# Denominator's sum moved from VectorE to GpSimd, and the column sums of w_out made in two lots

## What is computed

```python
for t in range(S):                                   # 4 batches, 8 heads, 768 steps, head_dim 48
    state = alpha[:, :, t, :, None] * state + einsum('bhd,bhe->bhde', k[:, :, t], v[:, :, t])
    y[:, :, t] = einsum('bhd,bhde->bhe', q[:, :, t], state)
x = y as 3072 tokens x 384

h = x @ w_in                                         # 384 -> 2048
P = a[0] + a[1]*h + a[2]*h*h + a[3]*h*h*h
Q = 1.0 + abs(b[0])*abs(h) + abs(b[1])*h*h
x2 = (P / (Q + 1e-06)) @ w_out                       # 2048 -> 384

h = x2 @ w_in2                                       # 384 -> 1024
solu = h * softmax(h)
ln = (solu - mean(solu)) / sqrt(var(solu) + 1e-06) * g_ln
out = ln @ w_out2                                    # 1024 -> 384
```

## Time and profile before

| what | us |
|---|---|
| median of 3 runs | 802.56 |
| lowest and highest | 801.42, 802.93 |
| the profiled execution, device time | 799.91 |
| its span, first to last instruction | 798.1 |
| PE busy | 773.5 (97%) |
| PEld busy | 720.8 (90%) |
| DVE busy | 688.1 (86%) |
| ACT busy | 593.4 (74%) |
| POOL busy | 303.9 (38%) |
| chain that ended last: PE, DVE, ACT | 68%, 14%, 9% |

### The profile page before, as it was taken

The page is one execution under the profiler, slowest core; times in us unless marked ns, Lnnn a source line. Parts: engine busy times, 40 slices in busy tenths (PEclk is TensorE's granted clock), DMA queues, the critical chain, the costliest instruction groups (busy, mean ns, idle before and its releaser), DMA issues.

```text
span 798.1 us, 16327 instructions
## 1 busy us (share of the span) xinstructions
PE 773.5 (97%) x5406; PEld 720.8 (90%) x5406; DVE 688.1 (86%) x1251; ACT 593.4 (74%) x1214; POOL 303.9 (38%) x405
## 2 busy tenths in 40 slices
PE   7999999799899999999999999999999999999998
PEld 6777778698799999999999999999999999999988
DVE  6999999799998898889888988898889888988854
ACT  6777778688877786778677867787778777877743
POOL 4999998122223232323232323232323232323211
PEclk9999999999999999999999999999999999999999
DMA  8999999200100010001000000000000000000000
GB/s 190 220 244 261 240 248 255 66 1 1 31 1 1 10 41 11 1 12 39 10 0 14 35 10 0 21 28 10 0 35 14 10 0 10 11 11 6 5 21 30
DMA packets 93542, 42.96 MB, mean 54 GB/s; under 512 B 80632, under 2 KB 90432, under 8 KB 93504
## 3 DMA queue, kind: packets, MB, share of 16 engines
q1 hardware_dynamic: 88944, 28.92, 15.2%
q0 software_dynamic: 4560, 13.57, 5.8%
HBM read 33.04 MB, written 9.44 MB: 53 GB/s over the span
## 4 chain that ended last, share of the span: by engine, by line
PE 68%; DVE 14%; ACT 9%; issue 4%; DMA 2%; SPq 1%; ACTq 0%; DVEq 0%; POOL 0%
PE h_ps L1172 18%; PE acc_ps L1198 18%; PE y_ps L1154 12%; PE z_ps L1216 12%; PE chunks_ring L337 2%; DVE work L1416 2%; PE z_ps L1226 2%; DVE rec L1408 2%; DVE den L1404 2%; DMA chunks_kin<-in_k_dram 2%; ACT rec L1305 1%; ACT g_hi L1295 1%; DVE chunks_kp L624 1%; DVE chunks_err L617 1%; DVE chunks_rec L620 1%
## 5 line engine op out<-in xcount | busy, mean ns | idle before, releaser
L1355 POOL TENSOR_TENSOR g_lo<-work,g_hi 128x384 fp32r<-128x384 f32 x128 | 130.8, 1022 | 401.5 <-ACT g_hi L1295 401.5
L1172 PE MATMUL h_ps<-x,w 128*128 (+1 forms) x1143 | 224.8, 340 | 6.0 <-DVE work L1426 4.4
L1198 PE MATMUL acc_ps<-g_hi,w 128*128 128x384 f32 x768 | 218.3, 338 | 2.3 <-POOL g_lo L1355 2.3
L1172 PEld LDWEIGHTS h_ps<-x,w 128*128 128x128 f32 x1143 | 200.5, 188 | 12.3 <-DVE work L1426 8.5
L1198 PEld LDWEIGHTS acc_ps<-g_hi,w 128*128 128x128 f32 x768 | 141.2, 188 | 2.8 <-POOL g_lo L1355 2.8
L1267 ACT ACTIVATE h<-h_ps 128x384 f32<-128x384 f32 x128 | 61.7, 482 | 98.9 <-PE h_ps L1172 98.8
L1198 PE MATMUL acc_ps<-g_lo,w 128*128 128x384 f32 x384 | 129.7, 338 | 0.0
L1421 DVE SCALAR_TENSOR_TENSOR den<-h,ncoef,den 128x384 f32<-128x384 f32 x128 | 78.6, 614 | 39.9 <-ACT den L1270 39.0
L1216 PE MATMUL z_ps<-w,x 128*128 128x512 f32 x396 | 99.9, 397 | 2.4 <-DVE lnT L1438 2.4
L1154 PE MATMUL y_ps<-w,lnT 128*128 128x384 f32 x528 | 99.9, 338 | 0.0
L1295 ACT ACTIVATE g_hi<-work 128x384 fp32r<-128x384 f32 x128 | 68.1, 532 | 38.2 <-DVE work L1416 35.0
(11 more groups left out here) (162 smaller groups left out, 1120.8 us busy)
## 6 DMA issues: line engine op xcount, KB each, us to landing
chunks_kin<-in_k_dram SPq DMA_DIRECT2D x32, 144.0 KB, 3.7
chunks_vin<-in_v_dram SPq DMA_DIRECT2D x16, 288.0 KB, 4.7
wstage<-in_moe_w_in_dram POOLq DMA_DIRECT2D x9, 512.0 KB, 5.0
attention_out<-solu SPq DMA_DIRECT2D x64, 72.0 KB, 3.1
out_dram<-ysb SPq DMA_DIRECT2D x24, 192.0 KB, 1.8
work<-in_alpha_dram SPq DMA_DIRECT2D x30, 144.0 KB, 4.3
chunks_qin<-in_q_dram POOLq DMA_DIRECT2D x28, 144.0 KB, 4.8
x<-attention_out SPq DMA_DIRECT2D x7, 576.0 KB, 3.9
```

Source lines behind the costliest of these rows:

```text
L1172: mm = nc.tensor.matmul(h_ps[:, s % 2, 0:TT], w1[:, wz, kc, s * P:(s + 1) * P], xs[:, xz, kc, :], start=(n == 0), stop=(n == 3 * KC - 1))
L1198: mm = nc.tensor.matmul(acc_ps[:, dc, 0:TT], w2[:, wz, f, dc * P:(dc + 1) * P], rhs, start=(f == 0 and n == 0), stop=(f == FC1 - 1 and n = ...
L1355: nc.gpsimd.tensor_tensor(g_lo[:, 1 - o, :], gate[:, 1 - o, :], g_hi[:, 1 - o, :].bitcast(F32), ALU.subtract).then_inc(glo_done, 1)
```

## The change

The sum of the denominator becomes a plain addition of two tiles and moves to GpSimd, at the head of its step. For that ACT's Square is scaled by the square root of |b1|, so that `h2` holds |b1| h*h. The root is made before the loop: ACT takes the absolute value in the attention's pair 14, GpSimd raises it to 0.5 behind the last weights and signals `coef_ready`, which is now what GpSimd waits for before the main loop. DVE's operation in each step goes, with its wait for `hw_ready`, and so do DVE's max (L1451) and wait ahead of the loop. The 16 matmuls of the column sums leave steps 2 to 9 of tile 0 and stand, eight and eight, behind h in steps 1 and 2.

```diff
@@ -515,6 +519,10 @@
                                      accum_out=seen[:, 3, bass.ds(n, 1)]).then_inc(ksq_seen, 1)
             if stage1(n):
                 squares_of_v(n, p, i + o)
+            if i_is(n, NPAIR - 2):
+
+                act.wait_ge(over.coef_loaded, 32)
+                nc.scalar.activation(over.b1_size, over.b1, ACT.Abs).then_inc(over.b1_size_done, 1)
             if i_is(n, NPAIR - 1):
 
                 act.wait_ge(x0_loaded, 16)
...
@@ -721,7 +729,7 @@
             nc.gpsimd.tensor_tensor(onehot[:], ident[:, 0:HB], ident[:, HB:P], ALU.add).then_inc(zeroed, 1)
             pool.wait_ge(zeroed, 5)
         pool.wait_ge(w_lo, over.w_pieces)
-        pool.wait_ge(neg_done, 1)
+        pool.wait_ge(coef_ready, 1)
         pool.sem_inc(joined, 1)
 
     def sync(sp):
...
@@ -863,6 +871,8 @@
         ident = sb("ident", [P, P])
         coef = sb("coef", [P, 6])
         ncoef = sb("ncoef", [P, 6])
+        half = sb("half", [P, 1])
+        b1_size = sb("b1_size", [P, 1])
         gln = sb("gln", [P, FC2])
         fits = sb("fits", [1, 1], mybir.dt.int32)
         work = sb("work", [P, 2, 2, TT])
...
@@ -878,6 +888,7 @@
         wstage = sb("wstage", [P, 2, 1024], F32, phase_a)
         coef_loaded = sem("coef_loaded")
         neg_done = sem("neg_done")
+        b1_size_done = sem("b1_size_done")
         coef_ready = sem("coef_ready")
         w_loaded = [sem(f"w_loaded{j}") for j in range(2)]
         w_scaled = sem("w_scaled")
...
@@ -950,13 +961,17 @@
                     nc.gpsimd.dma_start(stage(j + 2), pieces[j + 2][0]).then_inc(w_loaded[j % 2], 16)
             pool.wait_ge(coef_loaded, 32)
             nc.gpsimd.tensor_scalar(ncoef[:], coef[:], -1.0, None, ALU.mult).then_inc(neg_done, 1)
+            nc.gpsimd.memset(half[:], 0.5).then_inc(neg_done, 1)
+            pool.wait_ge(neg_done, 2)
+            pool.wait_ge(b1_size_done, 1)
+            nc.gpsimd.tensor_tensor(ncoef[:, 5:6], b1_size[:], half[:], ALU.pow).then_inc(coef_ready, 1)
 
 
         over = Handover(work[:], x, w1, h_ps, att_stored, x0_loaded, xhi_done, x_ready, h_ready, att_copied, judged, g_ln, gln[:], gln_ready,
-                        len(list(weight_pieces())))
+                        len(list(weight_pieces())), coef[:, 5:6], b1_size[:], coef_loaded, b1_size_done)
         with phase_a:
             chunks = attention_by_chunks(nc, ctx, q, k, v, alpha, scratch, ident, fits, prepare_weights, homes, w_lo, solu[:], over)
-        scan, joined = attention_by_scan(nc, ctx, q, k, v, alpha, scratch, ident, fits[:], w_lo, neg_done, solu[:], over)
+        scan, joined = attention_by_scan(nc, ctx, q, k, v, alpha, scratch, ident, fits[:], w_lo, coef_ready, solu[:], over)
 
 
         x2 = sb("x2", [P, 2, KC, TT], F32R)
...
@@ -1173,15 +1188,15 @@
                                                           xs[:, xz, kc, :], start=(n == 0), stop=(n == 3 * KC - 1))
                                     n += 1
                             mm.then_inc(h_ready, 1)
-                        if i_is(i, 0) and 2 <= s < FC2 + 2:
-
-                            fc = s - 2
-                            if fc == 0:
+                        if i_is(i, 0) and s in (1, 2):
+
+                            if s == 1:
                                 pe.wait_ge(share_ready, 1)
-                            for z in (HI, LO):
-                                mm = nc.tensor.matmul(y_ps[:, 0:DM], share, w4[:, z, fc, :], start=(fc == 0 and z == HI),
-                                                      stop=(fc == FC2 - 1 and z == LO))
-                            if fc == FC2 - 1:
+                            for fc in range(FC2 // 2 * (s - 1), FC2 // 2 * s):
+                                for z in (HI, LO):
+                                    mm = nc.tensor.matmul(y_ps[:, 0:DM], share, w4[:, z, fc, :], start=(fc == 0 and z == HI),
+                                                          stop=(fc == FC2 - 1 and z == LO))
+                            if s == 2:
                                 mm.then_inc(means_summed, 1)
                         if s == 3:
                             last_product(i, s)
...
@@ -1264,7 +1279,7 @@
                             act.wait_ge(h_ready, g + 1)
                             if not (i_is(i, 0) and s == 0):
                                 act.wait_ge(den_ready, g)
-                            nc.scalar.activation(h2[:], hp, ACT.Square)
+                            nc.scalar.activation(h2[:], hp, ACT.Square, scale=ncoef[:, 5:6])
                             if not (i_is(i, 0) and s < 2):
                                 act.wait_ge(g_done, g - 1)
                             nc.scalar.activation(den[:, o, :], hp, ACT.Abs, scale=coef[:, 4:5]).then_inc(hw_ready, 1)
...
@@ -1327,6 +1342,11 @@
                 def body(i):
                     for s in range(FC1):
                         o = s % 2
+                        g = chunk(i, s, 0)
+                        if g is not None:
+
+                            pool.wait_ge(hw_ready, g + 1)
+                            nc.gpsimd.tensor_tensor(den[:, o, :], h2[:], den[:, o, :], ALU.add).then_inc(den_ready, 1)
                         t = block_at(i, s, GAINS)
                         if t is not None:
                             pool.wait_ge(squares_done, t + 1)
...
@@ -1417,9 +1437,6 @@
                                                            op0=ALU.add, op1=ALU.mult).then_inc(g_done, 1)
                         if g is not None:
 
-                            dve.wait_ge(hw_ready, g + 1)
-                            nc.vector.scalar_tensor_tensor(out=den[:, o, :], in0=h2[:], scalar=ncoef[:, 5:6], in1=den[:, o, :],
-                                                           op0=ALU.mult, op1=ALU.add).then_inc(den_ready, 1)
                             dve.wait_ge(num0_done, g + 1)
                             nc.vector.tensor_tensor(num[:, o, :], num[:, o, :], h_ps[:, o, 0:TT], ALU.mult).then_inc(num1_done, 1)
                             dve.wait_ge(num1_done, g + 1)
...
@@ -1448,8 +1465,6 @@
                                                            op0=ALU.mult, op1=ALU.add).then_inc(ysb_ready, 1)
                         if FC1 - KC >= s > FC1 - 2 * KC and (not isinstance(i, int) or i < NT - 1):
                             x_lo(i + 1, s - (FC1 - 2 * KC + 1))
-                nc.vector.tensor_tensor(ncoef[:, 5:6], coef[:, 5:6], ncoef[:, 5:6], ALU.max).then_inc(coef_ready, 1)
-                dve.wait_ge(coef_ready, 1)
                 rounds(dve, body)
 
 
```

## The result

The changed kernel took 813.05 us (median, 812.56 to 813.68), the kernel before beside it on the same chip 801.99: a ratio of 1.0138, with a 95% interval of 1.0121 to 1.0156. The change costs 11 us. The profiled execution of after spans 811.2 us against 798.1, so 13.1 more, and that difference is the one taken apart here.

The account below looks back on a forecast made before the run. Bound: tile 0's VectorE-ScalarE loop, 3.56 us a turn, then TensorE with z stalls. Turns +1.0, first chunk +0.5, hand-over -0.5 and stalls +1.05 gave +2.0, so 804.6 us; range 800.5 to 816.

Parts of the forecast that it names:

- the first rival: GpSimd's add, once reading, shuts VectorE out in tile 0 and before z stalls: turn 4.01, +13.0 us, 815.6; chance 0.27.
- the forecast: VectorE's reciprocal and gate hold GpSimd's add, lengthened to 1.49, in tile 0: +2.0 us, 804.6; chance 0.38.
- The turn: One round of tile 0's VectorE and ScalarE loop, 3.56 us before; predicted 3.63 as the add delays Ln.
- Thirteen ordinary turns: Tile 0 loop, errors 0 to 9 and 13 to 17: 13 x 0.08 = +1.0 us.
- the means turn: The turn with the copy of the means: g_hi, means and Ln queue behind the gate, so 0.
- The three turns with x conversion: Turns of 3.89 us with VectorE already full: 0 expected; first rival +0.2 each.
- The first chunk: Nothing overlaps there, so GpSimd's longer add and hand-overs make Ln 0.52 us later; bounds 0.4 and 0.6.
- The hand-over to tile 1: acc at 219.10 waited 2.27 us, taken for L1432; one VectorE operation fewer ahead gives -0.54.
- The stalls: Seven TensorE waits before the z product, mostly one a tile: +0.15 us each, +1.05 together; bounds 0 and +5.6.
- The column sums, Abs, memset and pow: Column sums moved in tile 0, and preparation before the loop: hidden by waits or idle time, all 0.
- Square's scale: ScalarE's Square scaled by an SBUF value: +0.09 us a chunk; bounds 0 and 0.10.
- The second rival: No contention worth the name in tile 0, add 1.02 to 1.1, turn 3.45: -1.9 us, 800.7; chance 0.22.

Follow-up runs that it names:

- experiment 1: Kernel before with only the column sums moved to steps 1 and 2 of tile 0: 802.06 us, ratio 1.0011.
- experiment 3: Kernel after with the plain denominator addition done by VectorE in the old place, not by GpSimd: 799.11 us, ratio 0.9970.
- the width of 96 columns: Kernel after with GpSimd's add over only the first 96 of 384 columns: 798.19 us, ratio 0.9950.
- experiment 2: Kernel after with the column sums back in steps 2 to 9: 814.71 us, ratio 1.0161.
- experiment 8: Kernel after with GpSimd's add also waiting for the gate of the chunk before, beside PSUM-reading products: 816.10 us, ratio 1.0178.
- experiment 9: Kernel after with ScalarE's Ln and Exp ahead of g_hi in each step: 826.58 us, ratio 1.0296.
- the copy of 5: Kernel before plus an unused GpSimd copy of 768 columns, one input, in each step of tile 0: 808.79 us, ratio 1.0071.
- the 192 columns of 6: Kernel after with GpSimd's add over only the first 192 of 384 columns: 803.38 us, ratio 1.0011.
- experiment 4: Kernel before plus a GpSimd add of weight columns, result unused, in each step of tile 0: 811.51 us, ratio 1.0117.
- experiment 7: Kernel after with the add on VectorE in tile 0 and on GpSimd from tile 1 on: 805.80 us, ratio 1.0042.
- experiment 10: Experiment 3 with ScalarE's copy of the column means moved from step 10 to step 3, behind Exp: 798.51 us, ratio 0.9959 of the kernel before.
- the memset of 5: Kernel before plus an unused GpSimd memset of 1,024 columns, no input, in each step of tile 0: 801.89 us, ratio 1.0008.

## Why the prediction was right and wrong

The time came out slower and inside the stated range, but near its upper end and by the first rival, not by the forecast (804.6). The case held likeliest was wrong in its mechanism.

- **The step that failed:** "VectorE shuts GpSimd out to its end, and isn't longer itself. So the reciprocal holds the add [...] it stands still until +2.36". It is the other way round when the add is first. The add ran on (1.04, not 1.49) and the gate was held (1.18, not 0.62). The row I built on, L1351 held to the end of L1404, had a VectorE operation that was first; L1337 beside L1416 reads a single element. Both are true and neither shows a GpSimd read of some length that starts first. The forecast took one side of a lock for a priority of one engine. Order decides: in the stall's chain the add is 0.10 ahead of the reciprocal and holds it, and where the gate is 0.15 ahead of the add, the add is held (1.34). The Trainium skill (SBUF — State Buffer, section "SBUF: two separate sides") has this rule, whoever starts first holds the pair, with two SBUF inputs on VectorE's side and only against a GpSimd operation that reads SBUF. The traces agree at each point: 1.18 for the gate, 0.62 beside a memset, 0.55 and 0.61 for PSUM readers.
- **When the hold ends:** the forecast let the gate's data begin 0.10 after its start, a term for which it names no row and that no run shows. The kernel after shows 0.40 to 0.43 from GpSimd's end to the end of each held operation, whether it takes 0.56 or 0.62 by itself. If the hold lasts to GpSimd's recorded end, "for the whole instruction" as the Trainium skill's section has it, the first 0.15 to 0.21 of such an operation need no shared port; that is an estimate, 0.56 and 0.62 less 0.41. The add's own start is alike: with 0.47 of the gate left it grew by 0.32, with 0.17 left by 0.02, so about its first 0.15 ran beside the gate.
- **The turn:** forecast 3.63, rival 4.01, measured 4.00. Thirteen ordinary turns cost 6.1 (rival 5.9), the means turn +0.58 (rival +0.55). The three turns with x conversion cost 1.4 and not the rival's 0.6: there the gates were 0.62, 1.43 and 1.19, and a reciprocal of 1.42 followed in the turn after.
- **The first chunk:** +0.5 expected, +0.47 measured. Right.
- **The hand-over to tile 1:** -0.54 in the forecast, nothing in the rival, +0.04 measured.
- **The stalls:** forecast +0.15 each; the wait went from 0.40 to 1.21, the rival's +0.80, and all seven by 5.5 us where the rival had 5.4.
- **The column sums, Abs, memset and pow:** 0 expected; experiment 1 shows the sums at 0 (T 645.1 against 645.0), experiment 3 the rest together. The forecast's own figures put the end of h of step 2 at 155.4 (153.09 + 0.5 + 1.84) and not 155.2, which changes nothing, since its Square started only at 157.84 in the kernel after.
- **Square's scale:** 0.57 long as expected, with 0.46 from its start to Abs's, and no harm in experiment 3.
- **The second rival** (turns 3.45, 1.9 us faster) is what the width of 96 columns gives: 3.43. Its condition was a GpSimd operation that doesn't meet the gate, and this one does.
- **The match of 13.1 with the rival's 13.0 is partly luck.** Its two terms were about right in size (8.6 for 7.6, 5.5 for 5.4); beside them stand three things that no case had: +1.6 from TensorE's clock, +0.4 from the attention stage, and about -3 from faster matmul work between the stalls.

## What to carry to other kernels

Before work is moved to GpSimd, list VectorE's operations that read two SBUF tiles and may start while GpSimd reads: here each was held until the GpSimd instruction was over and ended 0.4 us behind it, whatever tiles that instruction touched. Taking the sum off VectorE freed 0.53 us a step of its queue, and the 1.04 us add on GpSimd cost 0.57 on the loop; moving it beside PSUM readers only made it late. A lock seen from one side tells nothing of who goes first; look for a row with the other order before building on it. When one instruction is moved, ask what else of that queue moves with it.

## What the runs showed of the hardware

- A GpSimd copy with one SBUF input of 0.95 us held the gate to 0.99; a memset of 0.95 left it at 0.62.
- In the kernel after, 60 VectorE operations held by a GpSimd operation of two SBUF inputs ended 0.40 to 0.43 us behind it, and 50 GpSimd adds that started with 0.27 us or more of such a VectorE operation left took 1.15 to 1.34 and not 1.02.
- TensorE's granted clock fell to 0.50 around the hand-over to tile 1 in half of the fourteen profiles: after and experiments 2, 3, 8 and 9, the copy of 5 and the 192 columns of 6, with waits ahead of acc of 2.71, 2.72, 2.19, 2.88, 2.78, 2.26 and 2.31. It stayed at 1.00 in before, 1, 4, 7, 10, the memset of 5 and the 96 columns of 6, with waits of 2.27, 2.25, 2.27, 2.69, 2.21, 2.25 and 2.13. So the length of that wait alone doesn't decide it, and what does is open. It is no fixed trait of a kernel either: the mean clock was 1.000 in three executions of the copy of 5, and 0.998 in the profiled one. In after the fall lasted some 3.4 us (about 229.5 to 232.9) and cost about 1.6.
- A tile's remainder without its z stall is 78.8 us in before and in experiments 1, 4 and 5, and 78.3 to 78.6 in the versions of after, whichever engine adds, but for experiment 9 (80.0), where TensorE has other waits. The same matmuls are a few nanoseconds shorter each (y_ps 338 and 336 ns). The column sums don't do it (experiment 1); whether the scaled Square or the missing VectorE operation does was not tried, and it stays open.
- The first error lay up to 3.2 us later (153.06 to 156.30) between profiled executions that differ only in later steps. A part of that is TensorE's clock in the attention stage. It fell to 0.50 at 12 to 14 us into the span, until about 19 us in experiments 4 and 7 and the 192 columns of 6 (first errors at 156.30, 155.95 and 156.13), and for about half as long in 2, 8, 10 and the memset of 5 (155.47, 155.87, 154.85 and 154.25). In the other seven it stayed at 1.00 there (153.06 to 154.45). What makes it fall, and the rest of the spread, are open. Windows of experiment 4 and then of before:

```profile
14.00:16.00 2.00, 2.00 (x18) 1.78 (x17) 0.23 (x1) 0.00 (x0) 0.23 (x1) 0.50 0.92 136
```

```profile
14.00:16.00 2.00, 2.00 (x26) 1.69 (x25) 1.78 (x2) 1.37 (x3) 0.11 (x1) 1.00 1.10 151
```

Executions of one kernel differ in the same way: 23 of the kernel before, taken beside experiment 7, have mean clocks from 0.992 to 1.000 and times from 799.65 to 808.64. This is inside every ratio above, which is why T is given.
